# Attention followed by two MLPs: operand splits per pair of heads with DMA copies, one addition per value product, transposed probabilities in two groups

## The reference

```
scores = scale * q @ k.T                      # per head, 576 x 576
cum    = cumsum(max(s, 0))
scores = where(causal, -1e9, scores + minimum(-(cum_i - cum_j), 0))
attn   = exp(scores - rowmax) / (rowsum + 1e-9)
x      = attn @ v                             # heads joined: 2304 x 512
h      = x @ w_in;  solu = h * softmax(h);  ln = layernorm(solu) * g;  x2 = ln @ w_out
y      = max(x2 @ w1, x2 @ w2, x2 @ w3) @ moe2_w_out
```

## Time and profile before

| | |
|---|---|
| Time, median of 3 runs | 772.84 us (771.74 to 778.02) |
| Profiled execution | 775.42 us, span 773.3 us |
| TensorE busy, share of the span | 727.6 us, 94% |
| VectorE busy | 418.7 us, 54% |
| ScalarE busy | 328.3 us, 42% |
| GpSimd busy | 225.7 us, 29% |
| Mean granted TensorE clock | 0.993 |
| DMA | 45.28 MB, mean 59 GB/s |

### The profile page before, as it was taken

The page is one execution under the profiler, slowest core; times in us unless marked ns, Lnnn a source line. Parts: engine busy times, 40 slices in busy tenths (PEclk is TensorE's granted clock), DMA queues, the critical chain, the costliest instruction groups (busy, mean ns, idle before and its releaser), DMA issues.

```text
span 773.3 us, 12787 instructions
## 1 busy us (share of the span) xinstructions
PE 727.6 (94%) x4312; PEld 662.6 (86%) x4312; DVE 418.7 (54%) x766; ACT 328.3 (42%) x795; POOL 225.7 (29%) x240
## 2 busy tenths in 40 slices
PE   3898999899899899999999999999999999999997
PEld 2777788788787788989898989999989999899995
DVE  8999999999985675535444364513203123032120
ACT  2888888888784443423233243412112121121111
POOL 6756669878762631404040200000000000000000
PEclk9999999999999999999999999999999999999999
DMA  6465464545341110106100031000010000100101
GB/s 154 115 165 139 135 149 119 131 124 143 88 91 43 42 37 6 41 1 176 29 0 0 0 109 56 1 21 22 1 42 1 14 28 0 41 0 0 41 0 42
DMA packets 46580, 45.28 MB, mean 59 GB/s; under 512 B 22164, under 2 KB 37652, under 8 KB 46516
## 3 DMA queue, kind: packets, MB, share of 16 engines
q1 hardware_dynamic: 46548, 44.86, 22.2%
HBM read 39.43 MB, written 5.38 MB: 58 GB/s over the span
## 4 chain that ended last, share of the span: by engine, by line
PE 66%; DMA 8%; POOL 7%; DVE 6%; issue 6%; SPq 4%; ACT 2%; POOLq 0%; ACTq 0%
PE ps L600 10%; PE ps L602 10%; PE ps L601 10%; DMA qk_raw<-in_qk_dram 8%; PE ps L532 4%; PE ps L534 4%; PE ps L533 4%; PE ps L520 4%; PE ps L522 4%; PE ps L521 4%; PE ps L613 3%; PE ps L614 3%; PE ps L615 3%; POOL qk_b L671 2%; POOL v_hl L675 2%
## 5 line engine op out<-in xcount | busy, mean ns | idle before, releaser
L602 PE MATMUL ps<-x_lo,w_hi 128*128 (+1 forms) x432 | 144.4, 334 | 0.0
L600 PE MATMUL ps<-x_hi,w_hi 128*128 128x384 f32 x432 | 144.3, 334 | 0.0
L601 PE MATMUL ps<-x_hi,w_lo 128*128 128x384 f32 x432 | 144.3, 334 | 0.0
L783 ACT ACTIVATE probs<-ps,nmax 128x576 f32<-128x576 f32 (+4 forms) x160 | 82.7, 532 | 14.2 <-DVE nmax L1002 14.2
L793 ACT ACTIVATE pt_hi<-ps 128x512 fp32r<-128x512 f32 (+1 forms) x128 | 69.7, 570 | 35.3 <-PE ps L432 32.6
L414 PE MATMUL ps<-k_a,q_a 128*128 128x288 f32 (+2 forms) x192 | 70.0, 369 | 12.9 <-DVE q_a L995 12.3
L432 PE MATMUL ps<-ident,probs 128*128 128x128 f32 x480 | 74.6, 285 | 7.7 <-DVE pt_lo L1009 3.1
L600 PEld LDWEIGHTS ps<-x_hi,w_hi 128*128 128x128 f32 x432 | 81.1, 188 | 0.2
L601 PEld LDWEIGHTS ps<-x_hi,w_lo 128*128 128x128 f32 x432 | 81.1, 188 | 0.2
L602 PEld LDWEIGHTS ps<-x_lo,w_hi 128*128 128x128 f32 x432 | 81.1, 188 | 0.0
L1009 DVE TENSOR_TENSOR pt_lo<-ps,pt_hi 128x512 fp32r<-128x512 f32 (+1 forms) x128 | 77.9, 649 | 3.4 <-ACT pt_hi L793 2.2
(11 more groups left out here) (102 smaller groups left out, 1469.1 us busy)
## 6 DMA issues: line engine op xcount, KB each, us to landing
qk_raw<-in_qk_dram SPq DMA_DIRECT2D x64, 288.0 KB, 4.3
rinvB<-rsum_dram SPq DMA_DIRECT2D x24, 192.0 KB, 4.0
stage<-in_moe_w_dram SPq DMA_DIRECT2D x18, 256.0 KB, 4.2
out_dram<-stage SPq DMA_DIRECT2D x18, 256.0 KB, 2.0
v_raw<-in_v_dram SPq DMA_DIRECT2D x32, 128.0 KB, 2.4
stage<-in_moe_w_out_dram SPq DMA_DIRECT2D x14, 256.0 KB, 2.7
stage<-in_moe_w_in_dram SPq DMA_DIRECT2D x4, 512.0 KB, 3.3
aux_dram<-setup SPq DMA_DIRECT2D x1, 576.0 KB, 4.6
```

Source lines behind the costliest of these rows:

```text
L600: pe.matmul(dst, w_hi[f][:, i, c, :], x2_hi[par][:, c, :], start=(c == 0), stop=False)
L601: pe.matmul(dst, w_lo[f][:, i, c, :], x2_hi[par][:, c, :], start=False, stop=False)
L602: mm = pe.matmul(dst, w_hi[f][:, i, c, :], x2_lo[:, c, bass.ds(g * GT, GT)], start=False, stop=(c == KC - 1))
L783: act.activation(dst, SCORES[c], ACT.Exp, bias=nmax[par][:, c:c + 1], accum_out=sums_all[:, c, bass.ds(t, 1)]).then_inc(exp_done, 1)
```

## The change

- **No padding.** Chunk 0 is now 64 rows wide and the others 128, with nothing in between (`first_of`, `chunk_offset`). Blocks that touch chunk 0 have 64 rows or columns.
- **Splits.** The queue loads q and k of two heads at once as 128 rows (`load_qk`). GpSimd scales q (`scale_q`), makes the high parts of q and k in one instruction (`qk_high`) and the low parts in another (`qk_low`), once per pair of heads. The queue then copies the parts from `split` into each head's `oper` with three DMAs of 64 rows (`copy_high`, `copy_low`), and loads the bias rows. VectorE's `q_low` is gone. `split_v` is wholly on GpSimd. For pair 0 the work is shared by GpSimd (k), ScalarE (high part of q) and VectorE (its low part).
- **Values.** The two halves are 288 columns each; one `copy_vlo` and one `add_parts` take the place of two.
- **Transposes.** Two groups instead of four: 8 blocks (960 columns) and 7 blocks (896 columns), each over the two banks 3 and 4. The second group waits until the low part of the first is done.
- **Order.** VectorE: maximum of chunk 4, addition, low part of group 0, maxima of chunks 3, 0, 1, 2, low part of group 1. ScalarE: high part of group 0, exponentials of chunks 4 and 3, high part of group 1, exponentials of chunks 0, 1, 2, copy of the values' low rows.
- The memsets of padding go; those of `sums_all` and `rinvT` move ahead of the cumulative sums on VectorE, with one of a part of PSUM bank 4.

```diff
     GROUPS = [
-        ([(2, 2), (2, 3), (2, 4), (0, 0)], J2),
-        ([(0, 1), (0, 2), (0, 3), (0, 4)], J0 + P),
-        ([(1, 1), (1, 2), (1, 3), (1, 4)], J1),
-        ([(4, 4), (3, 3), (3, 4)], J4),
+        ([(2, 2, PAD), (2, 3, PAD + P), (2, 4, PAD + 2 * P), (0, 0, BANK - PAD),
+          (0, 1, BANK), (0, 2, BANK + P), (0, 3, BANK + 2 * P), (0, 4, BANK + 3 * P)], J2, PAD, 2 * BANK),
+        ([(1, 1, 0), (1, 2, P), (1, 3, 2 * P), (1, 4, 3 * P), (4, 4, BANK), (3, 3, BANK + P), (3, 4, BANK + 2 * P)],
+         J1, 0, 7 * P),
     ]
...
+            def copy_high(h, pb):
+                rows = slice(D * h, D * (h + 1))
+                sp.dma_start(f32(oper[h][0:D, 0:2, :]), split[rows, pb, 0:2, :]).then_inc(oper_loaded[h], 16)
+            def copy_low(h, pb):
+                rows = slice(D * h, D * (h + 1))
+                sp.dma_start(f32(oper[h][D:P, 0:2, :]), split[rows, pb, 0:4:3, :]).then_inc(oper_loaded[h], 16)
+                sp.dma_start(f32(oper[h][0:D, 2:4, :]), split[rows, pb, 1:3, :]).then_inc(oper_loaded[h], 16)
...
             load_qk(0, 0)
+            load_qk(1, 1)
             load_v(0, 0)
-            load_qk(1, 1)
-            sp.wait_ge(rows_zeroed, 2)
+            load_v(1, 1)
+            sp.wait_ge(k0_hi_ready, 1)
+            sp.wait_ge(q0_hi_ready, 1)
+            copy_high(0, 0)
+            sp.wait_ge(k0_lo_ready, 1)
+            sp.wait_ge(q0_lo_ready, 1)
+            copy_low(0, 0)
             sp.wait_ge(cum_ready, 1)
...
+            copy_high(1, 0)
+            copy_low(1, 0)
             sp.dma_start(aux_dram, setup[:, :, :]).then_inc(aux_stored, 16)
...
+            def reload_qk(pair, pb):
+                sp.wait_ge(oper_loaded[0], pair * 64 - 64)
+                sp.wait_ge(oper_loaded[1], pair * 64 - 64)
+                load_qk(pair, pb)
+            def refill(pair, h, pb):
+                t = 2 * pair + h
+                if h == 0:
+                    sp.wait_ge(lo_ready, pair)
+                    sp.sem_inc(sp_passed, 1)
+                sp.wait_ge(scores_done, 3 * (t - 1))
+                copy_high(h, pb)
+                copy_low(h, pb)
+                load_aux(t, h)
+            def reload_pair(pair, pb, known=None):
+                if known is None or known + 2 < PAIRS:
+                    reload_qk(pair + 2, pb)
...
+                refill(pair + 1, 0, 1 - pb)
+                if known != 0:
+                    reload_v(2 * pair + 1, 1)
+                refill(pair + 1, 1, 1 - pb)
+                reload_v(2 * pair + 2, 0)
...
             def turn(g, t, par, known):
                 if g == 0:
                     pe.wait_ge(exp_done, NCH * t)
-                    if known != 1:
-                        pe.wait_ge(pt_lo_done, 4 * (t - 1) - 1)
-                elif g >= 2 or known != 1:
-                    pe.wait_ge(pt_lo_done, 4 * (t - 1) + g - 1)
+                if g == 1 or known != 1:
+                    pe.wait_ge(pt_lo_done, 2 * (t - 1) + g)
...
+            def qk_low(pair, pb):
+                pool.wait_ge(hi_ready, pair)
+                raw = split[:, pb, 2:4, :]
+                pool.tensor_tensor(raw.bitcast(F32R), raw, split[:, pb, 0:2, :], ALU.subtract).then_inc(lo_ready, 1)
```

ScalarE's slot:

```diff
             def slot(t, par, known):
                 if live(known, 1):
                     pt_high(0, t, par, known)
-                    split_v(t - 1, 1 - par, None if known is None else known - 1)
-                    pt_high(1, t, par, known)
                 if live(known, 0):
                     exp(t, par, known, 4)
                     exp(t, par, known, 3)
                 if live(known, 1):
-                    pt_high(2, t, par, known)
-                    pt_high(3, t, par, known)
+                    pt_high(1, t, par, known)
                 if live(known, 0):
                     exp(t, par, known, 0)
+                    exp(t, par, known, 1)
                     exp(t, par, known, 2)
-                    exp(t, par, known, 1)
                 if live(known, 2):
-                    copy_vlo_a(t, par, known)
-                    copy_vlo_b(t, par, known)
+                    copy_vlo(t, par, known)
```

VectorE's slot:

```diff
             def slot(t, par, known):
-                if live(known, -1):
-                    q_low(t + 1, 1 - par)
                 if live(known, 0):
                     row_max(t, par, 4)
-                    row_max(t, par, 0)
-                    row_max(t, par, 3)
                 if live(known, 3):
-                    add_a(t, par, known)
+                    add_parts(t, par, known)
                 if live(known, 1):
                     pt_low(0, t, par, known)
-                    pt_low(1, t, par, known)
                 if live(known, 0):
+                    row_max(t, par, 3)
+                    row_max(t, par, 0)
                     row_max(t, par, 1)
-                if live(known, 3):
-                    add_b(t, par, known)
-                if live(known, 0):
                     row_max(t, par, 2)
...
                 if live(known, 1):
-                    pt_low(2, t, par, known)
-                    pt_low(3, t, par, known)
+                    pt_low(1, t, par, known)
```

More of the change, by code:

```diff
@@ L18, with first_of @@
 MASKED = -1.0e9
+def first_of(c):
+    return 0 if c == 0 else P * c - P // 2
 def chunk_offset(c):
-    return P * c * (c + 1) // 2
+    return sum(first_of(i + 1) for i in range(c))
 def attention_and_mlp(nc, qkT, v, s, w_in, w_out, g_ln, w1, w2, w3, w_out2, out):
-    HEADS, D, _, S = qkT.shape
+    PAIRS, _, _, S = qkT.shape
+    HEADS, D = 2 * PAIRS, P // 2
     DM, FF = w_in.shape
@@ L46, in attention_and_mlp @@
     NCH = (S + PAD) // P
-    SP = S + PAD
     SCALE = float(D) ** -0.5
@@ L189, in attention_and_mlp @@
         qk_loaded = [sem(f"qk_loaded{i}") for i in range(2)]
-        aux_loaded = [sem(f"aux_loaded{i}") for i in range(2)]
+        sp_passed = sem("sp_passed")
+        oper_loaded = [sem(f"oper_loaded{i}") for i in range(2)]
         v_loaded = [sem(f"v_loaded{i}") for i in range(2)]
         w_loaded = sem("w_loaded")
[L193 to L196, removed]
+        k0_hi_ready = sem("k0_hi_ready")
+        q0_hi_ready = sem("q0_hi_ready")
+        k0_lo_ready = sem("k0_lo_ready")
+        q0_lo_ready = sem("q0_lo_ready")
+        q_scaled = sem("q_scaled")
+        hi_ready = sem("hi_ready")
+        lo_ready = sem("lo_ready")
         v_hi_ready = sem("v_hi_ready")
@@ L284, in _, with load_qk @@
             sp.dma_start(s_sb, s).then_inc(s_loaded, 16)
[L286 to L291, removed]
+            def load_qk(pair, pb):
+                sp.dma_start(split[:, pb, 2:4, :], qkT[bass.ds(pair, 1)].rearrange("a p i s -> (a p) i s")).then_inc(qk_loaded[pb], 16)
@@ new lines, in _ @@
+            reload_pair(0, 0, 0)
+            reload_pair(1, 1, 1)
+            with sp.Fori(1, 1 + KC // 2) as quad:
+                for i in range(2):
+                    pair = 2 * quad + i
+                    reload_pair(pair, i)
+                    sp.dma_start(stage[:, bass.ds(pair * FF - 2 * FF, FF)], w_in[bass.ds(pair * P - 2 * P, P), :]).then_inc(w_loaded, 16)
+            with sp.Fori(1 + KC // 2, 1 + KC // 2 + FB // 2) as quad:
+                for i in range(2):
+                    pair = 2 * quad + i
+                    reload_pair(pair, i)
+                    sp.dma_start(stage[:, bass.ds(pair * DM + KC * FF - (2 + KC) * DM, DM)],
+                                 w_out[bass.ds(pair * P - (2 + KC) * P, P), :]).then_inc(w_loaded, 16)
@@ L1039, in _ @@
-            q_low(0, 0)
-            for i in range(2):
-                dve.memset(v_raw[i][0:PAD, 0, :], 0.0)
-                for c in range(NCH):
-                    dve.memset(probs[i][:, chunk_offset(c):chunk_offset(c) + PAD], 0.0)
-            dve.memset(sums_all[:, :, :], 0.0)
-            dve.memset(rinvT[:, :, :], 0.0).then_inc(setup_dve, 1)
+                dst = flat[D * (1 - par):D * (2 - par), bass.ds(columns(t, par, known), S)].rearrange("p (a b) -> p a b", a=2)
+                dve.wait_ge(vlo_copied, t - 2)
```

311 lines of the change are left out of this document (132 added, 179 removed).

## The result

The kernel after takes 835.08 us (median of 4 runs, 832.90 to 846.06), the kernel before 773.19 in the same session (4 runs): ratio 1.078, 95% interval 1.072 to 1.084. 780 was forecast, within 768 to 794. The side was right, the size was not: +62 us where the sum had +7.6. The ratio leaves out the run of 846.06, which is over 1.5% above the fastest. The profiled execution took 832.9 us, its span is 831.0, 57.7 more than before.

A forecast was written before the change was run, and what follows sets the result against it. VectorE's list was taken to bound a head now, a ring of dependent steps after. Heads +1.2, start +6.6, slot 28 -0.7, end +0.5 sum to +7.6 us: 772.84 becomes 780.4, called 780; range 776 to 786, with rivals 768 to 794.

The forecast's parts named there:

- ring for VectorE's list: Attention heads: dependent steps replace VectorE's list as limit, 6.85 us for 6.80, +1.2 over 24 heads; slot 28 gives -0.7.
- the ring: Dependent steps from one turn(0) to the next, across TensorE, ScalarE and VectorE: sum 6.90 us a head, taken as 6.85.
- the start: Before the first score: later low part of q, then two copies; first score at 17.4 us, +5.1.
- About 250 [GB/s] at a full share: Queue's DMA in a head: 1.48 MB at the rate of the earlier windows takes 5.9 us of 6.85.
- Hidden, with about 1 us to spare: Operand copies of a head: wanted some 8.4 us after they can start, so they cost no time.
- Rival 2: Copies bind: at 180 GB/s a head's DMA takes 7.2 us, ending at 791; at 160 it ends at 805. Chance 0.25.
- The turning: Eight transposes opening a head on TensorE: 1.06 us; four loading 64 columns of weights could save up to 0.1.
- Rival 1: Faster: a head falls below 6.5 us; 765 at 6.35 a head, 757 at TensorE's own 6.1. Chance 0.17.
- GpSimd: Its splits for a pair of heads: about 3.0 us of low parts, the rest under 7, hidden in 13.7.
- the 1.5 us of head 2: Head 2's copies land at about 29 us, wanted at 27.9: about 1.5 us late, bounds 0 and 3.5.
- The end: Slot 32: turn(1) stands behind the low part of group 0, +0.5 us (0 to 1).

The follow-up runs named there:

- 9: Kernel after with half of each operand copy, chunk 0's block onto itself put first and transposed from 128 rows instead of 64: 783.12 us, ratio 1.010.
- 2: Kernel after, each of a head's three operand copies moving half its columns from head 2 on: 795.85 us, ratio 1.028.
- Experiment 1: Kernel before with six batches of six 288 KB DMAs ahead of its first load: SBUF copies 192 to 388 GB/s, HBM loads 218 to 329.
- Experiment 8: Kernel after with half of each operand copy and every transposed block 128 columns wide: 798.1 us, ratio 1.032.
- 10: Kernel after with half copies, chunk 0's own block transposed from 128 rows, and key block 0's values also taken over 128 rows: 785.12 us, ratio 1.015.
- 6: Kernel after with four transpose groups in the order of the kernel before, and half of each operand copy: 794.31 us, ratio 1.025.
- 7: Kernel before with its own operands and padding, but two transpose groups, joint addition and the new order: 795.26 us, ratio 1.028.

## Why the prediction was wrong

The 30 intervals, profiled executions, step by step (numbers in brackets are experiments):

| | us | forecast |
|---|---|---|
| before | 207.4 | |
| ring for VectorE's list, wide rows (9) | 208.9: +1.5 | +1.2, -0.7 |
| the 64-row block (2 against 9) | 216.0: +7.1 | -2.4 to 0 |
| slow first three heads (after against 2) | 221.8: +5.8 | 0 |
| copies too slow, late operands, half clock (after against 2) | 257.4: +35.6 | 0 |
| start, to the first turn(0) | +5.3 | +5.1, and 1.5 behind it |
| last interval and what lies behind | +2.4 | +0.5 |

The kernel is slower, as forecast, but of the 57.7 us of span the forecast's own terms, the ring and the start, give about 7.

- **The copies: the step that failed.** "About 250 [GB/s] at a full share: 1.48 / 0.25 = 5.9 us of 6.85" divided a window's rate by its share. That rate was an average over loads from HBM in the state of those windows, and carried over to copies within SBUF of which it held none. Experiment 1 gives them 192 to 208 GB/s; in the kernel after 1.48 MB at the 222 of 60 to 220 us is 6.7 us, 93% of an undisturbed head of 7.13 (86 to 97% by the two windows of 20 us), and while 512 KB of weights are loaded in a pair it is more. "Hidden, with about 1 us to spare" was the false step, and TensorE's waits for `oper`, up to 3.96 us, stood in its place. That is under 100%, and still some operands come late. The queue's own waits may be the reason: between 60 and 220 us its copies wait 16.5 us for scores, in 11 places, and its raw loads 7.3 us for earlier transfers. No run took these waits away, so this part is argued and not shown. The nearest row for an SBUF read, 576 KB in 4.6 us (128 GB/s), and the 6.9 us that the prediction worked out from the 196 GB/s of the Trainium skill (SBUF — State Buffer, "Door 1: The DMA port swizzle") both spoke against the value taken. Rival 2 had the mechanism, at 0.25 and too cheap.
- **Its price.** Rival 2 let a head grow to what the DMAs take, +0.35 us. The loss is not of that kind: behind the third head 15.5 us of waits in a few slots, and then TensorE at half clock for 58 us, 55 of them within the intervals, which is up to 27 us of work. The two make 43, more than the 35.6 of the step; part of the low clock lies inside the waits, where it costs nothing. Undisturbed heads were no longer for the copies, 7.13 with all of them and with half.
- **The slow start.** 5.8 us of the 41.4 between the kernel after and experiment 2 lie in the first three heads, where the granted clock reads 1.00 and the matmuls have the length of the lower one. No term of the forecast held it. Experiment 8 had it with half the copies and no late operand there, so it isn't shown to be the copies'; what brings it is open.
- **The turning.** "That could save up to 0.1" for narrow blocks was of the wrong sign: the one low block costs 0.21 (9), and the width gives 0.03 (8). All other terms of the ring were right to 0.05 us, and the ring as a whole, 6.90, stands at 6.92 once that block is gone (9, 10). TensorE's own work in a head was 19.5 of 20 us, not 18; it came out even with the ring.
- **The groups and the joint addition** neither win nor lose on the new operands (6). On the old operands they lose 20 us (7), where the ring meets a VectorE that still has the low part of q. Rival 1, heads under 6.5 us, came nowhere near.
- **GpSimd** is hidden: its wait for the raw data, 54 us, and its 192 us of work show slack.
- **The start** was right: first score at 17.80 for 17.4, first turn 5.3 us later for 5.1; the 1.5 us of head 2 came as a late operand of 1.17 us at 31.72, within the first three heads.
- **The end** is 1.9 us more than forecast, and was not followed up.

## What to carry to other kernels

Price a DMA by the rows it spans and by the memory it reads, from a row of the same kind, and where none exists give the slow value the greater chance when it fills the period: here a queue that needed some 93% of the period gave no steady slowdown but late operands now and then. Where the waiting engine's clock falls with the wait, a late operand costs more than its own length: here 15.5 us of waits cost 35.6. Check the granted clock against the length of a known matmul, since the two can disagree. And before an operand of fewer rows is put among full ones on TensorE, count the changes of height, not the rows saved.

## What the runs showed of the hardware

- A copy within SBUF between 64 rows and 64 rows: 192 GB/s into the same half, 208 into the other; over 128 rows 388.
- Loads from HBM that go to either half in turn from one queue (232 GB/s) are hardly faster than into one half (218).
- One transpose of 64 rows among seven of 128 makes their sequence 1.30 us instead of 1.09; a matmul of 64 rows and 288 columns follows its like after 0.24 us, one of 128 rows after 0.22 or, in a row of such, 0.13 to 0.14.
- After a wait of 3.96 us TensorE's lower clock held for nearly 18 us more with the engine busy all the time, after one of 3.52 us for 6, after one of 2.09 us for 18, and after one of 2.87 us in 11 for 4 us. What makes the difference was not settled.
- At the start of the kernel after, a matmul of 448 columns took 0.72 us at a granted clock that reads 1.00; the same took 0.72 at 0.50 and 0.45 in an undisturbed head.
